# Attention outputs in column halves, one padded scan for all head pairs, two sequences in turn, and a ramp of 2, 2, 4 units

## What is computed

```python
for t in range(S):
    state = alpha[:, :, t, :, None] * state + np.einsum('bhd,bhe->bhde', k[:, :, t], v[:, :, t])
    y[:, :, t] = np.einsum('bhd,bhde->bhe', q[:, :, t], state)
```

```python
h = x @ w_in                                            # first layer
g = np.maximum(h, 0.0) + alpha * np.minimum(h, 0.0)
x = g @ w_out
h = x @ w_in2                                           # second layer
g = np.where(h >= 1, h, np.where(h <= -1, 0.0, (h + 1) ** 2 / 4))
out = g @ w_out2
```

## Time and profile before

| | us |
|---|---|
| median of 3 runs | 977.68 (975.34 to 981.53) |
| the profiled execution | 981.99 |
| its span, first to last instruction | 980.3 |
| TensorE busy | 946.6 (97%), mean granted clock 0.977 |
| VectorE, GpSimd, ScalarE busy | 448.1, 354.8, 302.8 |

### The profile page before, as it was taken

The page is one execution under the profiler, slowest core; times in us unless marked ns, Lnnn a source line. Parts: engine busy times, 40 slices in busy tenths (PEclk is TensorE's granted clock), DMA queues, the critical chain, the costliest instruction groups (busy, mean ns, idle before and its releaser), DMA issues.

```text
span 980.3 us, 13041 instructions
## 1 busy us (share of the span) xinstructions
PE 946.6 (97%) x5050; PEld 815.9 (83%) x5050; DVE 448.1 (46%) x732; ACT 302.8 (31%) x561; POOL 354.8 (36%) x322
## 2 busy tenths in 40 slices
PE   7888999899999999999999999999999999999998
PEld 6877999889988888888888888888888888888886
DVE  4566546656555554455532444333333333333332
ACT  2323222222322232232224543233233332332322
POOL 5234333323223232222324764434334334343332
PEclk8777999999999999999999999999999999999999
DMA  5721113111311111112011320010010010100101
GB/s 162 212 46 33 33 34 63 35 33 33 65 33 33 33 33 33 33 37 49 13 65 32 97 66 1 1 33 1 1 33 1 0 33 1 33 1 1 32 1 33
DMA packets 21101, 37.02 MB, mean 38 GB/s; under 512 B 2160, under 2 KB 14448, under 8 KB 21040
## 3 DMA queue, kind: packets, MB, share of 16 engines
q1 hardware_dynamic: 21040, 36.19, 15.7%
HBM read 31.47 MB, written 4.72 MB: 37 GB/s over the span
## 4 chain that ended last, share of the span: by engine, by line
issue 43%; PE 32%; POOL 20%; DVE 3%; DMA 1%; SPq 0%; ACT 0%; POOLq 0%; DVEq 0%; ACTq 0%
POOL g_lo L303 16%; PE h_ps L670 4%; PE y_ps L670 4%; PE y_ps L672 4%; PE y_ps L671 4%; PE h_ps L672 4%; PE h_ps L671 4%; PE a_ps L640 2%; POOL x_lo L310 2%; POOL w_lo L283 2%; PE a_ps L616 1%; PE a_ps L636 1%; PE a_ps L628 1%; DVE prod L467 1%; DVE inv L474 1%
## 5 line engine op out<-in xcount | busy, mean ns | idle before, releaser
L303 POOL TENSOR_TENSOR g_lo<-g,g_hi 128x512 fp32r<-128x512 f32 (+2 forms) x208 | 251.7, 1210 | 507.5 <-ACT g_hi L391 503.9
L384 ACT ACTIVATE g<-h_ps 128x512 f32<-128x512 f32 (+2 forms) x208 | 117.6, 565 | 493.9 <-PE h_ps L672 475.4
L670 PE MATMUL y_ps<-g_lo,w_hi 128*128 128x512 f32 (+2 forms) x624 | 234.4, 376 | 8.9 <-POOL g_lo L303 8.8
L670 PE MATMUL h_ps<-x_lo,w_hi 128*128 128x512 f32 (+2 forms) x624 | 240.9, 386 | 0.1
L672 PE MATMUL h_ps<-x_hi,w_lo 128*128 128x512 f32 (+2 forms) x624 | 234.2, 375 | 0.0
L671 PE MATMUL h_ps<-x_hi,w_hi 128*128 128x512 f32 (+2 forms) x624 | 233.9, 375 | 0.0
L672 PE MATMUL y_ps<-g_hi,w_lo 128*128 128x512 f32 (+2 forms) x624 | 233.3, 374 | 0.0
L671 PE MATMUL y_ps<-g_hi,w_hi 128*128 128x512 f32 (+2 forms) x624 | 233.3, 374 | 0.0
L531 DVE SCALAR_TENSOR_TENSOR g<-g 128x512 f32<-128x512 f32 x96 | 66.4, 692 | 248.7 <-ACT g L384 248.7
L670 PEld LDWEIGHTS y_ps<-g_lo,w_hi 128*128 128x128 f32 x624 | 118.2, 189 | 30.8 <-POOL g_lo L303 6.5
L524 DVE SCALAR_TENSOR_TENSOR g<-g,slopes,h_ps 128x512 f32<-128x512 f32 (+2 forms) x112 | 74.8, 669 | 142.9 <-ACT g L384 142.3
(11 more groups left out here) (69 smaller groups left out, 565.7 us busy)
## 6 DMA issues: line engine op xcount, KB each, us to landing
qka_sb<-qka SPq DMA_DIRECT2D x44, 288.0 KB, 4.8
y_all<-w SPq DMA_DIRECT2D x16, 384.0 KB, 6.4
qka_sb<-w SPq DMA_DIRECT2D x16, 384.0 KB, 3.1
v_sb<-v SPq DMA_DIRECT2D x24, 192.0 KB, 5.1
y<-y_all SPq DMA_DIRECT2D x18, 256.0 KB, 2.4
qka_sb<-qka SPq DMA_DIRECT2D x4, 192.0 KB, 4.2
qka_sb<-qka SPq DMA_DIRECT2D x4, 96.0 KB, 3.0
slopes<-slopes_in SPq DMA_DIRECT2D x1, 8.0 KB, 4.8
```

The costliest lines, as they stand in the source:

```text
L303: nc.gpsimd.tensor_tensor(g_lo[:, s % G_RING, 0:w_], g32[:, s % G32_RING, 0:w_], g_hi[:, s % G_RING, 0:w_].bitcast(F32), ALU.subtract).the ...
L384: nc.scalar.activation(g32[:, s % G32_RING, 0:w_], h_ps[s % 2][:, 0:w_], ACT.Relu, scale=-1.0 if first else 0.5, bias=0.0 if first else 0. ...
L670: nc.tensor.matmul(out_, wh, lo, start=start, stop=False)
```

## The change

- The outputs are computed in halves of 64 tokens, which land on partitions 0 to 63 and 64 to 127, and the sums for each head apart (48 by 48). The outputs come ahead of the sums.
- The pairs' alphas lie behind one another with a zero ahead of each, and one scan over 516 columns does all four; where a pair starts, `starts` adds 1 and `ends` the reciprocal of the product. Alpha has its own tile and its own load, free when the inverse scan is done.
- Units alternate between two sequences, with two states.
- Decay is 4 steps ahead of the turn, scores 2, mix 1. VectorE does the decay behind `activate`, GpSimd the scaling behind `g_lo`.
- `FIRST` is 2, 2, 4, 4, 4, 4, 4.
- All splits of `w_lo` but the first three tiles go to VectorE, in one instruction over 768 columns; ScalarE and VectorE split tile f + 3 in step f.
- In the start VectorE scales the first q, GpSimd splits nothing ahead of the second, the mask of unit 1 goes into `g32`, and there are more idle matmuls. Loads are ordered anew; q and k are one transfer with the rows between filled by the host.

```diff
-FIRST = (2, 3, 3, 4, 4, 4, 4)
+FIRST = (2, 2, 4, 4, 4, 4, 4)
...
-EARLY = 4
+EARLY = 3
+SEG = CHUNK + 1
+SCAN = PAIRS * SEG
...
-        for _stage, _lag in (("decay", 5), ("scores", 3), ("mix", 1), ("turn", 0)):
+        for _stage, _lag in (("decay", 4), ("scores", 2), ("mix", 1), ("turn", 0)):
...
-WARM = 20
-FILL = {("scores", 0): 3, ("scores", 1): 1, ("mix", 0): 4, ("mix", 1): 2, ("turn", 1): 3}
+WARM = 24
+FILL = {("scores", 0): 8, ("scores", 1): 2, ("mix", 0): 2, ("turn", 0): 2, ("mix", 1): 3, ("turn", 1): 2}
...
+def place_of(u):
+    pair, w = divmod(u, 2 * CHUNKS)
+    return 2 * pair + w % 2, w // 2
...
+            def load_alpha(u):
+                if u >= 2:
+                    sp.wait_ge(inv_done, u - 1)
+                sp.dma_start(by_pair(alpha_sb[0:ROWS, u % 2, 0:SCAN])[:, :, 1:SEG], decays[u]).then_inc(alpha_loaded[u % 2], 16)
+            def load_v(u):
+                if u >= 2:
+                    sp.wait_ge(outputs_done, u - 1)
+                    ge(sp, state_summed, states_before(u - 1))
+                sp.dma_start(v_of(u), v[u]).then_inc(v_loaded[u % 2], 16)
...
@@ gpsimd
+            keep_last(0)
+            keep_last(1)
+            scale_q(1)
+            for i in range(EARLY):
+                split_in(i)
+                split_out(i)
...
+                    if s + 1 < STEPS:
+                        hidden_lo(s + 1)
                     for stage, u in plan_of(s):
                         if stage == "decay":
+                            keep_last(u)
                             scale_q(u)
-                    if s + 1 < STEPS:
-                        hidden_lo(s + 1)
-                    if n == 0 and f + EARLY < FT:
-                        split_in(f + EARLY)
...
@@ scalar
-            splits = {("decay", 1): [0, 1], ("scores", 0): [2], ("scores", 1): [3], ("turn", 0): [4], ("turn", 1): [5]}
+            splits = {("scores", 1): [0], ("turn", 0): [1], ("turn", 1): [2]}
...
-                    if n == 0 and f + 6 < FT:
-                        split_w(f + 6)
+                    if n == 0 and f + EARLY < FT:
+                        split_w(f + EARLY)
...
@@ vector
-                nc.vector.tensor_tensor(w_lo[:, i % FT, D_MODEL:], raw_of(i)[:, D_MODEL:],
-                                        w_hi[:, i % FT, D_MODEL:].bitcast(F32), ALU.subtract).then_inc(w_lo_out_done, 1)
+                nc.vector.tensor_tensor(w_lo[:, i % FT], raw_of(i), w_hi[:, i % FT].bitcast(F32),
+                                        ALU.subtract).then_inc(w_lo_done, 1)
...
-                for h in range(PAIRS):
-                    nc.vector.tensor_tensor_scan(prod[0:ROWS, h], al[:, h], zeros[0:ROWS], 1.0,
-                                                 ALU.mult, ALU.add).then_inc(prod_done, 1)
+                nc.vector.tensor_tensor_scan(prod[0:ROWS], al[:, 0:SCAN], starts[0:ROWS], 0.0,
+                                             ALU.mult, ALU.add).then_inc(prod_done, 1)
...
+                nc.vector.tensor_tensor_scan(inv[0:ROWS, ::-1], al[:, SCAN:0:-1], ends[0:ROWS, ::-1], 0.0,
+                                             ALU.mult, ALU.add).then_inc(inv_done, 1)
...
+                    activate(s + AHEAD)
+                    for stage, u in plan_of(s):
                         if stage == "decay":
                             decay(u)
-                    activate(s + AHEAD)
...
@@ tensor
+                halves = [slice(HALF * i, HALF * (i + 1)) for i in range(2)]
+                for h in range(PAIRS):
+                    if not fresh(u):
+                        for t in halves:
+                            nc.tensor.matmul(o[t, 2 * HD * h:2 * HD * (h + 1)], q[:, h, t], state[0:ROWS, u % 2, h],
+                                             start=True, stop=False)
+                    for e in range(2):
+                        c = slice((2 * h + e) * HD, (2 * h + e + 1) * HD)
+                        for t in halves:
+                            last = nc.tensor.matmul(o[t, c], att_of(u)[:, e, h, t], vs[:, c], start=fresh(u),
+                                                    stop=fresh(u) or e == 1)
+                last.then_inc(outputs_done, 1)
                 if keeps_state(u):
                     pe.wait_ge(k_tok_done, states_before(u) + 1)
                     for h in range(PAIRS):
-                        last = nc.tensor.matmul(scores_bank(u, 1)[0:ROWS, 2 * HD * h:2 * HD * (h + 1)], k_tok[:, h],
-                                                v_of(u)[:, 2 * HD * h:2 * HD * (h + 1)], start=True, stop=True)
+                        for e in range(2):
+                            r, c = slice(ODD * e, ODD * e + HD), slice((2 * h + e) * HD, (2 * h + e + 1) * HD)
+                            last = nc.tensor.matmul(sums[r, c], k_tok[:, h, r], vs[:, c], start=True, stop=True)
                     last.then_inc(state_summed, 1)
```

More of the change, by code:

```diff
@@ L15 @@
 ODD = 64
+HALF = 64
 ROWS = ODD + HD
@@ L47, with keeps_state, fresh, added_before @@
 FIRST_PLAN = [("decay", 0), ("decay", 1), ("scores", 0), ("scores", 1), ("mix", 0), ("turn", 0), ("mix", 1), ("turn", 1)]
-WARM = 20
-FILL = {("scores", 0): 3, ("scores", 1): 1, ("mix", 0): 4, ("mix", 1): 2, ("turn", 1): 3}
+WARM = 24
+FILL = {("scores", 0): 8, ("scores", 1): 2, ("mix", 0): 2, ("turn", 0): 2, ("mix", 1): 3, ("turn", 1): 2}
 def plan_of(step):
     return sorted(PLAN.get(step, []), key=lambda task: ORDER.index(task[0]))
+def place_of(u):
+    pair, w = divmod(u, 2 * CHUNKS)
+    return 2 * pair + w % 2, w // 2
+def keeps_state(u):
+    return place_of(u)[1] < CHUNKS - 1
+def fresh(u):
+    return place_of(u)[1] == 0
 def states_before(u):
-    return STATES * (u // CHUNKS) + min(u % CHUNKS, STATES)
-def keeps_state(u):
-    return u % CHUNKS != CHUNKS - 1
+    return sum(keeps_state(x) for x in range(u))
+def added_before(u):
+    return sum(keeps_state(x) and not fresh(x) for x in range(u))
 def block_of(u):
     return max(n for n in range(N1) if STARTS[n] <= u)
-def build_program(nc, qka, v, w, alpha, out):
+def build_program(nc, qk, decays, v, w, alpha, out):
     with ExitStack() as ctx:
@@ L111, in build_program @@
         stored = sem("stored")
-        pads_set = [sem(f"pads_set{i}") for i in range(2)]
+        pads_set = sem("pads_set")
+        starts_set = sem("starts_set")
         state_cleared = sem("state_cleared")
-        zeros_set = sem("zeros_set")
         ident_set = sem("ident_set")
@@ L727 @@
     from concourse.bass_utils import run_bass_kernel_spmd
+    units = [place_of(u) for u in range(UNITS)]
+    rows = [*range(HD), *range(ODD - HD), *range(HD, 2 * HD)]
     def heads_on_partitions(x):
         x = x.reshape(BATCH, PAIRS, 2, CHUNKS, CHUNK, HD).transpose(0, 3, 2, 5, 1, 4)
-        return x.reshape(UNITS, 2, HD, PAIRS, CHUNK)
+        x = x.reshape(BATCH, CHUNKS, 2 * HD, PAIRS, CHUNK)[:, :, rows]
+        return np.stack([x[b, c] for b, c in units])
     def weight_tiles(w_in, w_out):
@@ L737 @@
     arrays = {
[L738 to L740 removed]
+        "qk": np.ascontiguousarray(np.stack([heads_on_partitions(x) for x in (q, k)], axis=2)),
+        "decays": np.ascontiguousarray(heads_on_partitions(alpha)),
+        "v": np.ascontiguousarray(np.stack([
+            v[b, :, c * CHUNK:(c + 1) * CHUNK].transpose(1, 0, 2).reshape(CHUNK, D_MODEL) for b, c in units])),
         "w": np.ascontiguousarray(np.stack([weight_tiles(moe_w_in, moe_w_out), weight_tiles(moe2_w_in, moe2_w_out)])),
@@ L748 @@
     r = run_bass_kernel_spmd(nc, [arrays], core_ids=[0])
-    y = r.results[0]["y"]
+    y = r.results[0]["y"].reshape(D_MODEL, UNITS, CHUNK)
+    y = np.stack([y[:, u] for u in np.argsort([CHUNKS * b + c for b, c in units])], axis=1)
     return np.ascontiguousarray(y.reshape(D_MODEL, BATCH * SEQ).T)
```

243 lines of the change are left out of this document (123 added, 120 removed).

## The result

The changed kernel is slower: 1008.68 us (1002.91 to 1010.30 in 4 runs) against 976.51, a ratio of 1.031 (95% interval 1.025 to 1.037). Forecast were 953 us and a range of 936 to 988.

What follows compares the result with a forecast made beforehand. TensorE's own work was taken as the bound, with real gaps only in the ramp. Start 24.5, blocks 75, 69, 327 plus 2.4, 66 and 391.5 gave 955.4 us of span, 957.1 profiled, 953 median; range 936 to 988.

Steps and rivals of the forecast that it cites:

- Scores nearer the turn: TensorE's scores in steady blocks: wait for k of 0.4 us a unit, cancelled by x_lo waits (0.6) that go.
- The decay beside GpSimd: VectorE's decay: 3.4 us undisturbed, 4.7 beside GpSimd's scaling of q, 6.0 if g_lo gets in front too.
- Column halves: TensorE's state sums and outputs: paired halves overlap, 2.1 us against 3.39, 1.2 saved a unit.
- Both rivals that denied it: TensorE's halves: serial, nothing saved, 982 us, chance 0.12; or a 59 ns matmul floor, 995 us, chance 0.13.
- the second rival: TensorE's sums and outputs: 59 ns a matmul is a floor, each unit 0.55 us slower, 995 us; chance 0.13.
- One scan: VectorE's decay: one scan over all pairs takes 1.2 us, the inverse 1.3, undisturbed decay 3.4 against 3.95.
- Two sequences in turn: State updates: two units' time each, nothing gained in steady blocks, the wait in the start removed.
- mask: Score masking in steady blocks: hides behind 4.08 us of products, at no cost.
- Ramp: Second block, 256 wide with four units: scores wait 3.1 us for k, a unit takes 15.7, the block 69.
- Splits: First block: each tile's split is a closed chain of 3.8 us for a step of 2.13; the block takes 75.
- Start: Stretch before the first product: 24.5 us against 36.4, with the clock staying up; bounds 22.5 and 31.
- The third rival: First two blocks: split chain and late k keep the clock low, each loses another 10 us, 973; chance 0.15.

Runs made afterwards that it cites:

- kernel 5: The changed kernel with every q scaled by VectorE behind k instead of by GpSimd: 973.07 us, ratio 0.996 to the kernel before.
- kernel 1: The changed kernel with decay 5 steps ahead of the turn instead of 4: 956.10 us, ratio 0.981 to the kernel before.
- Kernel 6: The changed kernel with eight idle identity matmuls ahead of each unit's wait for k: 985.19 us, ratio 1.010 to the kernel before.
- kernel 4: The kernel before with only the outputs and sums in column halves: 947.94 us, ratio 0.972 to the kernel before.
- Kernels 3 and 9: First blocks of 2, 3, 3 units again: in the changed kernel, 1009.52 us; in the changed kernel with decay a step earlier and splits ahead, 939.85 us.
- kernel 7: The changed kernel with ScalarE's split four tiles ahead and VectorE's split at the beginning of its step: 987.44 us, ratio 1.013 to the kernel before.

## Why the prediction was wrong

It failed at one step, "Scores nearer the turn": "k is ready at 8.65 (up to 9.95)" and "I take a wait of 0.4 a unit (bounds 0 and 1.4)". The wait measured is 1.65 us (1.8 by the starts of the products), above the upper bound, and the prediction's own sign of being wrong, scores of steady units waiting over 1 us, came. TensorE's arrival was right (8.5 us after the turn for 8.55), and so was the start of the decay (3.90 for 3.95). Two things were wrong.

- The decay beside GpSimd was priced at 4.7 us, 6.0 at most. Measured are 6.36, and k is ready at 10.3. I had counted one or two GpSimd instructions in its way; there are three. The one left out is g_lo of the next step, which runs when the decay now starts, just behind the activation; in the earlier trace rows the product scans ran free, because the decay began elsewhere. The undisturbed pieces were right: 1.23, 0.2, 1.23, 0.69 us, 3.35 with the prediction's 3.4; the three collisions added 1.04, 1.01 and 0.88. Each of the three costs what is left of the GpSimd instruction when VectorE's would begin (1.18, 1.16 and 1.02 us), less 0.14. The rule of the Trainium skill that the prediction named (page "SBUF — State Buffer", section Who interferes with whom) says that the later of two such instructions waits for the whole of the other; all three agree with it but for these 0.14 us, and kernel 5 shows it by taking one partner away. The rule was applied to the neighbours in the old schedule and not to those in the new one.
- The clock was let stay up in these blocks. The prediction had charged it for the ramp only, where it was low before. Behind eight of the 15 waits in the third to sixth block it fell, and TensorE lost another 1.8 us or so each time: its busy time there is 340.0 us, against 325.7 in kernel 1, 14.3 more. Kernel 6 shows this term by itself, at 11.5 us net in these blocks and 18 of span with the second block.

Together the waits (24.7 us) and the clock (14.3) are 39 us in the third to sixth block, where the prediction let a wait of 0.4 a unit cancel against the old x_lo waits. The work beside them was 3.7 us less than forecast, which gives 329.4 + 39.0 - 3.7 = 364.7. With the 39 us alone the forecast would have been 992 instead of 953, on the right side of 977. The wait at k was in the plan's own arithmetic one step (4.1 us) from being nothing, as kernel 1 shows, and I had not asked what the step of lag bought.

The other steps, in their order:

- **Column halves**: right. 2.09 us against a computed 2.1 in a steady unit, 1.42 against 1.4 in a fresh one, 28 us against 29 in the whole (kernel 4). Both rivals that denied it fall: records begin 30 ns apart (32 from 15.20 to 16.16) and in the steady unit 28 (eight from 384.32 to 384.54), so 59 ns was no floor. By the Trainium skill's figure of about 62 ns a matmul, which its page "TensorE: Matmul & The Clock Gate" (section What happens when you issue a matmul) gives for a decoding mode with the hardware decoder off, the second rival would have held; records 28 to 30 ns apart show that this bound was not in force here. The Trainium skill's page "TensorEngine Tiling (Array Packing)", section Key Properties, says that different tiles load and multiply in parallel; the trace agrees, with the same 28 to 30 ns. The same section says that changing the tiling mode drains TensorE; the mix shows no more of it than the 0.15 us in the sum.
- **One scan**: 1.23 us for 1.2 and 1.3, right, but with three collisions in place of two the decay is as long as before. No run has the one scan without the rest of the change, so what it is worth by itself is not shown.
- **Two sequences in turn** and **mask**: no wait for a state or for masked scores is in the list of waits; right as far as that goes, but not timed by itself.
- **Ramp**: the second block 74.1 for 69. Scores did wait about 3 us for k, as forecast; a unit takes 17.6 us there (from the wait at 116.70 to that at 134.32) for the 15.7 computed, at a clock of 0.88. Kernels 3 and 9 show no cost of the ramp itself.
- **Splits**: the chain was right, 3.92 us for 3.8, and kernel 7 shows its cost, 16 us in the block. The block took 80.5 for 75. Its clock was 1.00 while the chain alone ran and fell behind the decays (0.76 from 46 to 60 us, behind a wait of 5.7, and 0.70 from 70 to 80), 0.88 in the mean; so I put the missing 5.5 us down to the clock, but no run separates this.
- **Start**: 23.4 for 24.5.

The third rival, the narrow ramp, came true in part: first and second block lost 10.6 us more than forecast, where it gave 20. It had the right mechanism, a late k and a low clock behind it, but I confined it to the 256-wide blocks, and most of the loss lies in the 512-wide ones.

## What to carry to other kernels

When a long piece of work is moved to another place in an engine's order, price it beside its new neighbours on the engine that holds it up, instruction by instruction, and compare its end with its user's arrival in the step in which it now stands. A wait on TensorE of a microsecond or two in an otherwise full stretch can cost more than itself, since a slow spell may follow. Here 24.7 us of waits of 1.65 brought 14.3 more at the low clock, and 18.3 us of waits of 1.1 to 1.6 (kernel 5) brought 3.4; so the price is a range, from the wait alone to about twice it. A change of many parts should be timed part by part: here one part brought 28 us, two others cost 53 and 21 (42 and 17 by the profiled spans), and the whole looked like a bad idea.

## What the runs showed of the hardware

Column halves do run together, also with float32 and weight tiles of 64 and 48 columns: records begin 28 to 30 ns apart with 48-column streams, 45 to 52 with 96-column ones (four from 384.54 to 384.72, four from 384.11 to 384.32). A scan over 516 columns in 112 partitions takes 1.23 us, in the reversed direction too, and 2.24 to 2.27 when a two-input GpSimd instruction of 1.2 to 1.3 us has begun just before it; that GpSimd instruction keeps its length, and one that began 0.79 us before the end of a scan was stretched by 0.56 us. The granted clock fell behind eight of 15 stands of 1.65 us, one of them with TensorE full for over 8 us ahead of it, and stayed up behind the other seven, behind four stands of 1.5 us, one in every 3.9 (the first block), and behind three of 1.76 us ahead of the products (kernel 1). When idle matmuls filled the stands, the clock of those blocks was 1.00.
